# Attention with pooled queries, then a channel mix: the queries' pair sums move from VectorE to GpSimd, and VectorE's first sum of key tiles moves later in pairs 9 to 13

## What is computed

```python
q_pool = q.reshape(B, H, S // 2, 2, D).mean(axis=3)        # B=4, H=8, S=1152, D=64: 576 queries a head
scores = scale * np.matmul(q_pool, k.transpose(0, 1, 3, 2))
scores = scores - np.max(scores, axis=-1, keepdims=True)
attn = np.exp(scores)
attn = attn / (np.sum(attn, axis=-1, keepdims=True) + 1e-09)
out = np.matmul(attn, v)
...
x = out.transpose(0, 2, 1, 3).reshape(B, S // 2, H * D)    # 4 x 576 tokens of 512
xn = (x - mu) / np.sqrt(var + 1e-06) * g_ln
result = x + np.maximum(xn @ w_ch1, 0.0) @ w_ch2           # 512 -> 2048 -> 512
```

## Time and profile before

| what | value |
|---|---|
| median of 3 runs | 792.25 us (792.03 to 792.56) |
| the profiled execution | 791.6 us, span 789.8 us, so 1.8 us lie outside the span |
| PE busy | 781.0 us (99%) |
| DVE busy | 643.1 us (81%) |
| POOL busy | 436.4 us (55%) |
| ACT busy | 424.8 us (54%) |
| granted TensorE clock | 1.00 of full speed |

### The profile page before, as it was taken

The page is one execution under the profiler, slowest core; times in us unless marked ns, Lnnn a source line. Parts: engine busy times, 40 slices in busy tenths (PEclk is TensorE's granted clock), DMA queues, the critical chain, the costliest instruction groups (busy, mean ns, idle before and its releaser), DMA issues.

```text
span 789.8 us, 17026 instructions
## 1 busy us (share of the span) xinstructions
PE 781.0 (99%) x6398; PEld 654.4 (83%) x6398; DVE 643.1 (81%) x1010; ACT 424.8 (54%) x946; POOL 436.4 (55%) x338
## 2 busy tenths in 40 slices
PE   8999999999999999999999999999999999999998
PEld 6777778777777777778779899999999998999897
DVE  6987988878888989988799779898778898766655
ACT  4676566765566755667853446543345444233431
POOL 3899988888888889988887024411211431131100
PEclk9999999999999999999999999999999999999999
DMA  8566533665345653435331354213356212512212
GB/s 190 138 150 150 126 83 91 150 150 131 83 106 131 149 143 84 98 93 138 87 79 54 96 158 120 68 54 123 108 128 168 74 56 67 173 55 68 59 37 81
DMA packets 80433, 84.80 MB, mean 107 GB/s; under 512 B 47200, under 2 KB 62048, under 8 KB 76768
## 3 DMA queue, kind: packets, MB, share of 16 engines
q1 hardware_dynamic: 80192, 83.65, 41.1%
q10 hardware_dynamic: 160, 0.07, 0.0%
HBM read 74.25 MB, written 9.44 MB: 106 GB/s over the span
## 4 chain that ended last, share of the span: by engine, by line
PE 92%; DVE 5%; issue 1%; ACT 1%; POOL 0%; DVEq 0%; ACTq 0%; POOLq 0%
PE banks L1395 25%; PE banks L1384 20%; PE banks L803 16%; PE banks L792 14%; PE banks L736 5%; PE banks L790 4%; DVE pm L1120 2%; PE banks L1362 2%; PE banks L819 2%; DVE acc_end L1066 1%; PE banks L830 1%; PE banks L744 1%; PE banks L864 1%; PE banks L769 0%; DVE q_sums L611 0%
## 5 line engine op out<-in xcount | busy, mean ns | idle before, releaser
L639 POOL TENSOR_TENSOR acc<-acc,pT 128x576 f32<-128x576 f32 x160 | 237.3, 1483 | 23.2 <-ACT pT L995 0.4
L1395 PE MATMUL banks<-w2f,hT 128*128 128x512 f32 x858 | 211.6, 391 | 0.0
L995 ACT ACTIVATE pT<-banks 128x576 f32<-128x576 f32 x288 | 171.6, 659 | 36.5 <-PE banks L790 31.6
L1120 DVE TENSOR_REDUCE pm<-banks 128x2 f32<-128x1024 f32 x128 | 153.5, 1222 | 39.8 <-PE banks L736 38.0
L1395 PEld LDWEIGHTS banks<-w2f,hT 128*128 128x128 f32 x858 | 159.8, 188 | 28.3
L792 PE MATMUL banks<-qT,kT 64*128 64x288 f32 x1728 | 162.5, 298 | 1.9 <-DVE pm L1120 1.2
L792 PEld LDWEIGHTS banks<-qT,kT 64*128 64x128 f32 x1728 | 133.9, 184 | 17.0 <-DVE pm L1120 6.7
L803 PE MATMUL banks<-pT,vn 128*64 128x288 f32 x1152 | 145.9, 407 | 0.0
L1473 ACT ACTIVATE hT<-mid 128x384 fp32r<-128x384 f32 x88 | 46.2, 525 | 173.4 <-DVE mid L1540 172.8
L439 POOL TENSOR_TENSOR w_sums<-w_stage 128x256 f32<-128x256 f32 x22 | 17.4, 792 | 219.8 <-DMA w_stage<-in_moe_w_ch_dram 208.0
L1540 DVE TENSOR_TENSOR mid<-banks,mid 128x384 f32<-128x384 f32 x154 | 85.5, 555 | 54.1 <-PE banks L1384 48.8
(11 more groups left out here) (129 smaller groups left out, 960.5 us busy)
## 6 DMA issues: line engine op xcount, KB each, us to landing
q_in_rows<-in_q_dram SPq DMA_DIRECT2D x56, 284.0 KB, 6.7
k_in_rows<-in_k_dram SPq DMA_DIRECT2D x56, 284.0 KB, 5.2
w_stage<-in_moe_w_ch_dram SPq DMA_DIRECT2D x24, 512.0 KB, 4.6
w_stage<-in_moe_w_ch_dram SPq DMA_DIRECT2D x48, 256.0 KB, 2.7
vn<-in_v_dram SPq DMA_DIRECT2D x16, 576.0 KB, 5.2
tokens<-xn SPq DMA_DIRECT2D x18, 256.0 KB, 2.8
token_sums<-tokens SPq DMA_DIRECT2D x72, 64.0 KB, 2.6
out_dram<-x SPq DMA_DIRECT2D x15, 256.0 KB, 3.2
```

The costliest lines, as they stand in the source:

```text
L639: nc.gpsimd.tensor_tensor(total, pT[:, h % 2, 0] if kt == 1 else total, pT[:, h % 2, kt], ALU.add).then_inc(chained, 1)
L995: nc.scalar.activation(pT[:, h % 2, kt], pair_banks("S", n)[:, :, 0:HW], ACT.Exp, scale=SCALE).then_inc(exp_done, 1)
L1120: nc.vector.tensor_reduce(pm[:, at // GROUPS, :, at % GROUPS], src, AX.X, ALU.max).then_inc(max_taken, 1)
L1395: last = nc.tensor.matmul(banks[:, k % 2 * (CT // 2) + kk], hT[:, k, a, tokens], w2f[:, (2 * u + k // 2) % 4, b], start=p == 0 and k < 2 a ...
```

## The change

- GpSimd, not VectorE, sums the queries of pair j + 3, behind its two `add_rest` of pair j (`next_queries(j + 3)`). Step `s` is gone from all three lists of VectorE.
- `LATE` is `range(2, PAIRS - 2)`, that is pairs 2 to 13, so that pairs 9 to 13 use `VECTOR_LATE` too.
- GpSimd adds 1e-6 to the variances, in all three parts, and makes the shift by three small operations (half the negated mean, times the inverse deviation, doubled). VectorE's L268 and L1213 are gone.

```diff
-    VECTOR_STEPS = "m m m m m a m m m m e l c o Q K a q k s"
-    VECTOR_LATE = "m m m m m m m m m e l c o Q K a q k a s"
-    LATE = range(2, PAIRS - 7)
+    VECTOR_STEPS = "m m m m m a m m m m e l c o Q K a q k"
+    VECTOR_LATE = "m m m m m m m m m e l c o Q K a q k a"
+    LATE = range(2, PAIRS - 2)
...
-    VECTOR_0 = "l e m m c m e m m m l m m m m m c a Q K a q k s"
+    VECTOR_0 = "l e m m c m e m m m l m m m m m c a Q K a q k"
...
-        def variance_eps(n):
-            nc.vector.wait_ge(moments_ready, CT * (n + 1))
-            nc.vector.tensor_scalar_add(var_eps[:], moments[:, :, 1], 1e-6).then_inc(var_ready, 1)
-
         def inverse_deviation(n):
 
+            nc.gpsimd.wait_ge(moments_ready, CT * (n + 1))
+            nc.gpsimd.tensor_tensor(var_eps[:], moments[:, :, 1], eps[:], ALU.add).then_inc(var_ready, 1)
             nc.gpsimd.wait_ge(var_ready, n + 1)
             nc.gpsimd.tensor_tensor(rstd[:], var_eps[:], minus_half[:], ALU.pow).then_inc(rstd_ready, 1)
...
                 add_rest(2 * j + 1)
+                if j + 3 < PAIRS:
+                    next_queries(j + 3)
                 if j == PAIRS - 5:
                     inverse_deviation(0)
+                    nc.gpsimd.tensor_tensor(half_mean[:], moments[:, :, 0], minus_half[:], ALU.mult).then_inc(mean_ready, 1)
                     pool.wait_ge(mean_ready, 1)
                     pool.wait_ge(rstd_ready, 1)
-                    nc.gpsimd.tensor_tensor(shift[:], minus_mean[:], rstd[:], ALU.mult).then_inc(mean_ready, 1)
+                    nc.gpsimd.tensor_tensor(half_shift[:], half_mean[:], rstd[:], ALU.mult).then_inc(mean_ready, 1)
+                    pool.wait_ge(mean_ready, 2)
+                    nc.gpsimd.tensor_tensor(shift[:], half_shift[:], half_shift[:], ALU.add).then_inc(mean_ready, 1)
...
-                    elif op == "s" and j + 3 < PAIRS:
-                        dve.wait_ge(q_in, 64 * (j + 4))
-                        dve.wait_ge(kq_turned, j + 3)
-                        sum_queries(nc.vector, j + 3).then_inc(q_summed, 1)
...
-                    variance_eps(0)
-                    nc.vector.tensor_scalar_mul(minus_mean[:], moments[:, :, 0], -1.0).then_inc(mean_ready, 1)
```

More of the change, by code:

```diff
@@ L175, in pooled_attention_channel_mix @@
         rstd = sb("rstd", [128, CT])
-        minus_mean = sb("minus_mean", [128, CT])
+        half_mean = sb("half_mean", [128, CT])
+        half_shift = sb("half_shift", [128, CT])
+        eps = sb("eps", [128, CT])
         shift = sb("shift", [128, CT])
@@ L286, in normalize_first @@
             nc.scalar.wait_ge(rstd_ready, 1)
-            nc.scalar.wait_ge(mean_ready, 2)
+            nc.scalar.wait_ge(mean_ready, 3)
             wait(nc.scalar, xn_sent[kk % 2], 16 * (kk // 2))
@@ L620, in attention_gpsimd @@
             nc.gpsimd.memset(minus_half[:], -0.5).then_inc(half_made, 1)
-            pool.wait_ge(half_made, 1)
+            nc.gpsimd.memset(eps[:], 1e-6).then_inc(half_made, 1)
+            pool.wait_ge(half_made, 2)
             pool.wait_ge(zeros_made, 1)
@@ L1570, in next_tokens @@
                     moments_of(n)
-                    variance_eps(n)
                 if p in (2, 3, 4):
@@ L1606, in mix_vector @@
                     moments_of(1)
-                    variance_eps(1)
                 next_tokens(u)
```

## The result

The changed kernel took 794.08 us (median of 10 runs, 793.75 to 795.59) against 792.12 for the kernel before in the same comparison: a ratio of 1.0027, with a 95% interval of 1.0017 to 1.0037. It is about 2.0 us slower.

The account below looks back on a forecast made before the run. TensorE, busy 99%, was taken as the bound, with 24.38 us as a pair's floor. Gains of 1.68 us less 0.25 and 0.15 gave 1.28 us, so 792.25 became 790.97, say 791.0 us; range 790.2 to 792.3.

Parts of the forecast that it names:

- the channel mix is bound by TensorE alone: From 391 us on, TensorE was busy 30.00 of 30.00 us, so VectorE's savings there were worth nothing.
- the channel mix unchanged: Expected sign after the change: the channel mix, following attention, would keep its time.
- The slower one: Rival, 7%: shared-port waits cost 0.3 us in each of twelve pairs, 3.6 against 1.7 gained, giving 794.1 us.
- if the mix moves: One of three signs that would prove the prediction wrong: the channel mix changes; no size given.
- Pair 2: Attention pair of 24.97 us: removing VectorE's 1.97 us sum of queries brings it to the floor, gaining 0.59 us.
- Pairs 9, 10, 13: Attention pairs 0.15 us over the floor each: moving the early `acc_end` to the list's end gains 0.45 us.
- Pairs 11 and 12: Attention pairs 0.47 and 0.27 us over the floor: VectorE stays about 0.1 us late, gaining 0.64 us.
- the excess is VectorE being late with maxima, and nothing else: Claimed cause of the 1.78 us by which attention pairs 2 and 9 to 13 exceed the 24.38 us floor.
- Pair 1: Attention pair whose `acc_end` would wait for GpSimd's later add until 52.8 us: 0.25 us lost, bounds 0 and 0.4.
- Pairs 12 and 13: GpSimd enters these attention pairs late, so `acc_end` may delay the turned token tile: 0.15 us lost, bounds 0 and 0.4.
- L268 and L1213 leaving VectorE: Two small operations between statistics and maxima in pairs 11 and 12, taken as 0.1 of 1.87 us.

## Why the prediction was wrong

**What failed is a term that isn't in the sum.** The prediction says that "the channel mix is bound by TensorE alone" and expects "the channel mix unchanged". The first half holds. The second doesn't follow from it: the part of the change that declares three tiles for one was given no price at all, and it moved TensorE's operands. The missing term is +3.0 us, against a sum of -1.28. It is shown from both sides: 64 bytes of nothing cost the kernel before 2.8 us (2.9 in the mix of its trace), and with the tensors in their old places the changed kernel is 1.0 to 1.3 us faster than the kernel before. None of the rivals had it. The slower one gave 794.1 us, which is the measured number, but that is chance: it would have lost time in attention, which gained 1.07 us. The prediction's own sign, "if the mix moves", is the one that came.

**The rest of the sum came out near, in part by luck.** 791.0 was forecast, and the change in the old places measured 791.02. But the median of the kernel before was 792.49 in that comparison and not 792.25, and the traces give a gain of 1.0 us where 1.28 was forecast. The terms that follow add up to that: 1.56 us gained in pairs 2 and 9 to 13 where 1.68 was forecast, and 0.55 lost in pairs 1 and 14 where 0.40 was put on pairs 1, 12 and 13. From the profile of the changed kernel:

- Pair 2, forecast 0.59: it became 0.61 us shorter.
- Pairs 9, 10, 13, forecast 0.45 in all: 0.16, 0.17 and 0.16.
- Pairs 11 and 12, forecast 0.64 of 0.74: 0.46 in pair 11, nothing in pair 12. The 0.2 to 0.3 us of pair 12 were not VectorE's lateness in pair 11 handed on, as I had counted them, so "the excess is VectorE being late with maxima, and nothing else" was wrong. The chain runs through the same `pT` of ScalarE in both kernels, 3.81 us behind the start of the pair; what holds that was not tried. Before, and after:

```profile
321.13 0.66 ACT pT L995
320.56 0.66 ACT pT L1002
```

- Pair 1, forecast 0.25 longer: it became 0.27 us longer. The `acc_end` met GpSimd's add, and took 1.60 us against the 0.75 of the earlier trace rows. The chain of waits:

```profile
52.48 1.60 DVE acc_end L1073
54.08 1.15 DVE pm L1127
```

and GpSimd at that time, where the earlier trace rows had the add at 50.33:

```profile
50.65 1.42 POOL L612 TENSOR_TENSOR q_sums<-q_in_rows 128x576 f32<-128x576 f32 x1
52.03 1.43 POOL L641 TENSOR_TENSOR acc<-pT 128x576 f32<-128x576 f32 x1
```

  With the sum late in pair 1 too, 0.3 us came back.
- Pairs 12 and 13, 0.15 us for GpSimd's backlog: pair 13 did not become longer for it. GpSimd's small operations with the inverse deviation took 2.3 us behind its sum of queries in pair 11, where I had estimated 2.8 without a row for the small ones, and ahead of pair 14 it waited 1.50 us for ScalarE again, so the backlog was gone.
- Pair 14, for which the sum has no term, became 0.28 us longer: from pair 13's first multiplication by values to pair 14's it was 24.81 us, and 24.53 before. Its early `acc_end` took 1.81 us, and 1.52 before. I had looked only at the pairs whose list changes. The same loss stands in the run with the old list of late pairs and not in the one with VectorE's L268 and L1213 kept (24.83 and 24.54 us), so it goes with the small operations on GpSimd and not with the late sums. By what way they reach pair 14 was not tried.

**GpSimd** makes each sum in 1.43 us (forecast 1.44), its second `add_rest` fell from 1.80 to 1.41, and 0.57 us of idle time are left ahead of its next pair (forecast 0.5). End of pair 8:

```profile
239.07 1.41 POOL L650 TENSOR_TENSOR acc<-acc,acc_end 128x576 f32<-128x576 f32 x1 [0.76 <-DVE acc_end L1073]
240.43 1.43 POOL L612 TENSOR_TENSOR q_sums<-q_in_rows 128x576 f32<-128x576 f32 x1
242.44 1.42 POOL L641 TENSOR_TENSOR acc<-pT 128x576 f32<-128x576 f32 x1 [0.57 <-ACT pT L1002]
```

**One edit was undervalued.** I gave 0.1 us to L268 and L1213 leaving VectorE. For the kernel before that was about right: from the start of L268 to the next maxima it was 0.15 us. With the sum of queries on GpSimd it is worth 1.1 us, since the addition would wait for it. The Trainium skill, "SBUF — State Buffer", section "Who interferes with whom", lists `tensor_scalar` among the VectorE operations that can take the shared port pair, and the trace agrees, 1.33 us beside GpSimd's sum against 0.17 us without it. I had applied that section to `acc_end` alone.

## What the runs showed of the hardware

The time of a matmul depends on where its operands stand in SBUF, by up to 4 ns of 230 in the mean of a group. Moving `hT` by 64 bytes lengthened each group of nine by 0.034 us, moving `w2f` with `xf_more` shortened those of 12 by 0.010 and made all groups of a kind equal to 0.001 us. The time is a fixed property of the places: the mixes of the kernel before and of the changed kernel in the old places agree group by group within 0.001 us, though GpSimd's instructions stand at other moments.

The Trainium skill, "SBUF — State Buffer", section "Who interferes with whom", says that PE never waits on anyone and that only the shared port pair causes contention. Nothing here contradicts it, since a time that repeats so exactly speaks against contention with another engine, and the section says nothing on the place of an operand.

What slows TensorE is open. It is not a shift common to all (`hT` back in place gave 2.1 of 3 us), not the place within 128 bytes alone (the move by 128 changed the times too), not the distance of the two operands (moved together, they still changed), and not the operands of the group alone (groups that read no moved tensor changed too). Which bits of the address count, and whether the weight load or the moving operand is held, was not tried. Attention's matmuls, whose operands moved as well, showed nothing: pairs on the floor took 24.36 to 24.40 us in all places.

## What to carry to other kernels

A new tile, however small, moves every tensor allocated behind it, and on an engine that is busy for 99% of the time a shift of 64 bytes was worth more than the whole reordering (3.0 us against 1.0 to 1.3). So compare the addresses before and after a change, time the kernel before with the same shift, and allocate small tiles last or in one block. A shift can also gain: `w2f` 64 bytes higher gave 1.4 us. Where VectorE and GpSimd share work, the worth of an edit depends on what the other engine does at that moment: an addition of 0.17 us cost 1.33, and the gain of three edits was gone when the late sums or the small operations were left out.
